# The last 64 rows of a product as 64-row matmuls, two f tiles side by side on the two parts of the array

## What is computed

```python
# attention: y of shape (B, H, S, D) -> x of shape (1536, 320)
h = x @ w_in                                  # 320 -> 2048
g = np.maximum(0.01 * h, h)
x = g @ w_out                                 # 2048 -> 320
expert_idx = np.argmax(x @ w_gate, axis=1)    # 8 experts, up to 384 tokens in each
h = np.maximum(np.einsum('ecd,edf->ecf', disp, w1), 0.0)   # 320 -> 1024, by expert
y = np.einsum('ecf,efd->ecd', h, w2)                       # 1024 -> 320
out[i] = gate_w[i] * y[expert_idx[i], pos[i]]
```

## Time and profile before

| | us |
|---|---|
| median of 3 runs | 449.36 |
| lowest to highest | 449.0 to 451.3 |
| the profiled execution, its own time | 448.94 |
| its span, from the first to the last instruction | 447.2 |
| PE busy in the span | 419.4 |
| DVE, ACT, POOL busy | 266.3, 218.2, 183.2 |
| mean granted TensorE clock, share of full speed | 0.979 |

### The profile page before, as it was taken

How to read it: one execution, slowest core, us unless ns; L and a number is a source line. 1 busy time by engine, 2 the same in 40 slices (tenths; PEclk the granted TensorE clock), 3 DMA queues, 4 the chain that set the end, 5 groups by cost and what they waited for, 6 DMA issues and landing times.

```text
span 447.2 us, 8125 instructions
## 1 busy us (share of the span) xinstructions
PE 419.4 (94%) x3025; PEld 397.9 (89%) x3025; DVE 266.3 (60%) x549; ACT 218.2 (49%) x484; POOL 183.2 (41%) x183
## 2 busy tenths in 40 slices
PE   7979999999999999999999999699999999999990
PEld 4958999899899989899999995399999999999990
DVE  6796786856479746388543643365663756755220
ACT  5616647463444354352443332156754677665431
POOL 3763525511121302010478000617474868881613
PEclk8999999999999999999999998989999999999996
DMA  8999704403221410000450404382875578760001
GB/s 230 340 321 351 265 1 135 134 12 92 89 65 70 134 54 2 1 1 1 139 173 12 132 11 161 107 256 74 251 215 156 133 243 262 206 191 2 3 11 52
DMA packets 24377, 56.88 MB, mean 127 GB/s; under 512 B 4868, under 2 KB 9670, under 8 KB 24332
## 3 DMA queue, kind: packets, MB, share of 16 engines
q1 hardware_dynamic: 19132, 47.88, 34.6%
q0 software_dynamic: 2688, 6.56, 5.3%
q10 hardware_dynamic: 2512, 1.82, 1.2%
HBM read 50.03 MB, written 8.31 MB: 130 GB/s over the span
## 4 chain that ended last, share of the span: by engine, by line
PE 80%; DVE 7%; ACT 5%; issue 4%; DMA 2%; POOL 1%; SPq 0%; DVEq 0%; POOLq 0%; ACTq 0%
PE bank L1261 20%; PE bank L1267 10%; PE bank L1248 9%; PE bank L1249 8%; PE bank L1250 8%; PE bank L1252 4%; PE bank L1251 4%; PE bank L1161 4%; PE bank L1114 2%; PE bank L1297 2%; PE bank L1338 2%; PE bank L1144 1%; ACT ee L629 1%; DMA nat<-in_nat 1%; PE bank L1130 1%
## 5 line engine op out<-in xcount | busy, mean ns | idle before, releaser
L1043 DVE SCALAR_TENSOR_TENSOR gl<-bank,gh 128x384 fp32r<-128x384 f32 x64 | 35.6, 557 | 61.1 <-ACT gh L748 52.2
L728 ACT ACTIVATE tt<-bank 128x384 f32<-128x384 f32 x64 | 31.3, 489 | 77.8 <-PE bank L1252 77.8
L1261 PE MATMUL bank<-woh,gh 128*128 128x320 f32 x192 | 59.3, 319 | 3.1 <-ACT gh L734 1.5
L508 POOL TENSOR_TENSOR w2l<-w2r,w2h 128x640 fp32r<-128x640 f32 x28 | 43.9, 1570 | 40.4 <-ACT w2h L610 40.2
L748 ACT ACTIVATE gh<-bank 128x384 fp32r<-128x384 f32 x64 | 31.5, 492 | 59.0 <-PE bank L1267 52.3
L1025 DVE TENSOR_TENSOR gl<-g,gh 128x384 fp32r<-128x384 f32 x64 | 40.6, 634 | 32.7 <-ACT gh L734 32.5
L1017 DVE TENSOR_TENSOR g<-bank,tt 128x384 f32<-128x384 f32 x64 | 35.3, 552 | 39.6 <-ACT tt L728 39.0
L1261 PE MATMUL bank<-wol,gh 128*128 128x320 f32 x192 | 57.2, 308 | 0.0
L734 ACT ACTIVATE gh<-g 128x384 fp32r<-128x384 f32 x64 | 33.4, 523 | 44.3 <-DVE g L1017 44.3
L1248 PE MATMUL bank<-xh,wih 128*128 128x384 f32 x128 | 46.2, 361 | 0.5 <-DVE xh L823 0.5
L498 POOL TENSOR_TENSOR y<-hs,rec 128x320 f32<-128x320 f32 x11 | 8.9, 812 | 91.8 <-DVE hs L877 80.9
(11 more groups left out here) (196 smaller groups left out, 1054.5 us busy)
## 6 DMA issues: line engine op xcount, KB each, us to landing
w1r<-in_w SPq DMA_DIRECT2D x32, 384.0 KB, 4.7
w2r<-in_w SPq DMA_DIRECT2D x32, 320.0 KB, 3.4
qkt<-in_qk SPq DMA_DIRECT2D x12, 416.0 KB
ee<-gsc SPq DMA_DIRECT2D x9, 512.0 KB, 5.9
nat<-in_nat SPq DMA_DIRECT2D x12, 372.0 KB, 5.0
wir<-in_w_in SPq DMA_DIRECT2D x4, 768.0 KB, 12.6
wor<-in_w_out SPq DMA_DIRECT2D x4, 640.0 KB, 14.5
nat<-in_nat SPq DMA_DIRECT2D x12, 160.0 KB, 4.9
```

The source lines that it names most:

```text
L508: gp.tensor_tensor(lo, raw, hi.bitcast(F32), ALU.subtract).then_inc(s_lo2, 1)
L728: a.activation(tt[m % 2][:], ps_h[m % 2][:, 0:TM], ACT.Copy, scale=0.01).then_inc(s_t, 1)
L1043: ve.scalar_tensor_tensor(gl[m % 2][:], ps_h[m % 2][:, 0:TM], 0.0, gh[m % 2][:].bitcast(F32), ALU.max, ALU.subtract).then_inc(s_gl, 1)
L1261: mm(ab, gh[m % 2][:, cols], w[:, f, c0:c1], start=first and f == 0 and i == 0, stop=False, skip_group_check=True)
```

## The change

`hidden` treats steps in pairs of an even and an odd f. The even step makes its first seven matmuls as before; the eighth, lo weights by x_hi, takes partitions 0 to 63 alone. Right behind it a 64-row matmul on partitions 64 to 127 makes the same part for f + 1, into the other bank, and opens that bank's sum. The odd step then has seven matmuls and goes on with a sum already begun. Since partitions 64 to 127 of x_hi's third tile hold the lo part, x's hi part is needed there a second time: ACT copies it into a new tile `xr` before DVE puts lo in its place, and DVE waits for that copy (`s_xr`). The even step waits, ahead of its seventh matmul, until the other bank has been read: for `s_g` in the first MLP, for `s_gl` in the experts. The odd step waits for nothing at its start. The router's steps are moved so that those that use the bank's upper columns fall on even f. The zeroed tile moves into the place of the last token tile's x_hi, whose first copy waits for the transfer that reads the zeros.

```diff
+        xr = [sb(f"xr{i}", [P, TM], F32R) for i in range(2)]
+        zeros, _ = at("zeros", [P, DM], F32, r_x + (NTM - 1) * per_tile)
...
+            def x_hi_again(dst, src, s, sem_n):
+                act.wait_ge(s_xh, sem_n)
+                cols = slice(s * P, (s + 1) * P)
+                a.activation(dst[P - DR:P, cols], src[P - DR:P, 2, cols].bitcast(F32), ACT.Copy).then_inc(s_xr, 1)
+
             def x_hi(n):
                 act.wait_ge(s_yT, n + 1)
+                if n == NCH - SUB:
+                    act.wait_ge(s_zero, 16)
...
+                x_hi_again(xr[n // SUB % 2], xh[n // SUB], n % SUB, n + 1)
...
+                x_hi_again(xr[e % 2], xeh[e % 2], s, NCH + e * SUB + s + 1)
...
-                    if t >= 0 and f in (3, 4, 5):
-                        copy_x2t(t, (f - 3,))
+                    if t >= 0 and f in (3, 5, 7):
+                        copy_x2t(t, ((f - 3) // 2,))
...
+                dve.wait_ge(s_xr, sem_n)
                 ve.tensor_tensor(dst_h[64:128, 2, cols], src3[64:128, 2, :], dst_h[64:128, 2, cols].bitcast(F32),
                                  ALU.subtract).then_inc(s_xl, 1)
...
-                    if t >= 0 and f in (5, 6, 7):
-                        take_logits(t, f - 5, ps_h[m % 2][:, TM:TM + E])
-                    if t >= 0 and f == 11:
+                    if t >= 0 and f in (6, 8, 10):
+                        take_logits(t, (f - 6) // 2, ps_h[m % 2][:, TM:TM + E])
+                    if t >= 0 and f == 12:
                         take_ranks(t, ps_h[m % 2][:, TM:TM + SUB * E])
...
-            def hidden(m, wh, wl, f, x_hi, x_lo, nt):
-                if m >= 2:
+            def hidden(m, wh, wl, f, x_hi, x_lo, x_again, nt):
+                ts = slice(0, max(nt, 2) * P)
+                hb, other = ps_h[m % 2][:, ts], ps_h[1 - m % 2][:, ts]
+                even = f % 2 == 0
+                if even and m >= 2:
                     pe.wait_ge(s_gl, m - 1)
-                ts = slice(0, max(nt, 2) * P)
-                hb = ps_h[m % 2][:, ts]
                 for kt in range(2):
-                    mm(hb, wh[:, f, kt, :], x_hi[:, kt, ts], start=kt == 0, stop=False)
+                    mm(hb, wh[:, f, kt, :], x_hi[:, kt, ts], start=even and kt == 0, stop=False)
                     mm(hb, wl[:, f, kt, :], x_hi[:, kt, ts], start=False, stop=False)
                     mm(hb, wh[:, f, kt, :], x_lo[:, kt, ts], start=False, stop=False)
-                mm(hb, wh[:, f, 2, :], x_hi[:, 2, ts], start=False, stop=False)
-                mm(hb, wl[:, f, 2, :], x_hi[:, 2, ts], start=False, stop=True).then_inc(s_h, 1)
-
+                if even:
+                    if 1 <= m <= M2:
+                        pe.wait_ge(s_g, m)
+                    elif m > M2:
+                        pe.wait_ge(s_gl, m)
+                    mm(hb, wh[:, f, 2, :], x_hi[:, 2, ts], start=False, stop=False)
+                    mm(hb, wl[0:DR, f, 2, :], x_hi[0:DR, 2, ts], start=False, stop=True).then_inc(s_h, 1)
+                    mm(other, wl[P - DR:P, f + 1, 2, :], x_again[P - DR:P, ts], start=True, stop=False)
+                else:
+                    mm(hb, wh[:, f, 2, :], x_hi[:, 2, ts], start=False, stop=True).then_inc(s_h, 1)
```

More of the change, by code:

```diff
@@ L55, in mlstm_moe_kernel @@
         base = ((nc.sbuf_base + 31) // 32) * 32
-        room = (nc.sbuf_usable_end - base) // 32 * 32 - 64
+        room = (nc.sbuf_usable_end - base) // 32 * 32 - 32
         ctx.enter_context(nc.sbuf_tensor("arena", [P, room], mybir.dt.uint8))
@@ L170, in mlstm_moe_kernel @@
         wg = sb("wg", [P, KT, E], F32)
-        zeros = sb("zeros", [P, DM], F32)
         before = sb("before", [P, P], BF16)
@@ L271, in mlstm_moe_kernel @@
         s_rec, s_z, s_y, s_yT = sem("recip"), sem("z_ready"), sem("y_ready"), sem("yT")
-        s_xh, s_xl = sem("x_hi"), sem("x_lo")
+        s_xh, s_xl, s_xr = sem("x_hi"), sem("x_lo"), sem("x_hi_last_rows_again")
         s_h, s_t, s_g, s_gh, s_gl, s_acc = sem("mlp_h"), sem("mlp_t"), sem("mlp_g"), sem("g_hi"), sem("g_lo"), sem("mlp_acc")
@@ L743, in _ @@
                         store(t)
-                    if t >= 0 and f == 9:
+                    if t >= 0 and f == 11:
                         router(t)
@@ L1030, in _ @@
                         attention(n, k)
-                    if t >= 0 and f == 8:
+                    if t >= 0 and f == 10:
                         router(t, lgs[:])
-                    if t >= 0 and f == 9:
+                    if t >= 0 and f == 11:
                         count(t)
-                    if t >= 0 and f == 10:
+                    if t >= 0 and f == 13:
                         gates_of(t)
-                    if t >= 0 and f == 11:
+                    if t >= 0 and f == 12:
                         places(t)
-                    if t >= 0 and f == 12:
+                    if t >= 0 and f == 14:
                         gate_parts(t)
@@ L1347, in h_step @@
                         pe.wait_ge(s_lo1, f // 2 + 1)
-                    hidden(m, wih, wil, f, xh[t], xl[t], nt)
+                    hidden(m, wih, wil, f, xh[t], xl[t], xr[t % 2], nt)
                 else:
@@ L1354, in h_step @@
                         pe.wait_ge(s_lo1, NPM + NPE * e + f // 2 + 1)
-                    hidden(m, ew[e % 3][0], ew[e % 3][1], f, xeh[e % 2], xel[e % 2], nt)
+                    hidden(m, ew[e % 3][0], ew[e % 3][1], f, xeh[e % 2], xel[e % 2], xr[e % 2], nt)
             def acc_step(m, nt):
@@ L1378, in _ @@
                 t, f = m // FI - 1, m % FI
-                if t >= 0 and f in (5, 6, 7, 11):
+                if t >= 0 and f in (6, 8, 10, 12):
                     pe.wait_ge(s_gl, m - 1)
-                    if f == 11:
+                    if f == 12:
                         positions(t, ps_h[m % 2][:, TM:TM + SUB * E])
                     else:
-                        logits(t, f - 5, ps_h[m % 2][:, TM:TM + E])
+                        logits(t, (f - 6) // 2, ps_h[m % 2][:, TM:TM + E])
                 h_step(m, SUB)
@@ L1392, in _ @@
                     acc_step(m - 1, SUB)
-                if t >= 0 and f in (3, 4, 5):
-                    transpose_x2(t, f - 3)
+                if t >= 0 and f in (3, 5, 7):
+                    transpose_x2(t, (f - 3) // 2)
                 for n, k in tasks_at(m, 1):
```

## The result

The changed kernel takes 485.41 us (median of 4, 483.2 to 492.3) beside 450.33 of the kernel before; the ratio is 1.078 with a 95% interval from 1.072 to 1.084. (Ratios in this document leave out executions more than 1.5% above the fastest of their kernel, here the one of 492.3.) Forecast were 485 and a range of 475 to 496. The profiled execution took 483.20 us, its span is 481.4.

What follows compares the result with a forecast made beforehand. PE was taken to bound the first MLP and the experts, without slack. 448.94 + 16.2 (mode, saving included) + 19.6 (wait) = 484.7; with the runs' median .4 above, 485 us, range 475 to 496.

Steps and rivals of the forecast that it cites:

- Part 1: First layer, both stages: one matmul slot saved per pair of steps, 7.2 + 2.7 = 9.9 us.
- Part 2: 64-row matmuls among full ones on PE: mode changes cost 16.2 us net, the saved matmuls already included.
- way in: PE, full to half height: .27 us from the last 384-column full matmul's start to the load.
- open load: PE weight load not hidden beside the previous matmul: .10 us entering half height, .11 leaving.
- way out: PE, half to full height: .27 us taken for 384 columns, bounds .27 and .32.
- Part 3: New wait before even steps' seventh matmul: 19.6 us lost in the experts, nothing put down for the first MLP.
- the restart: PE resuming after the new wait in the experts: .05 + .08 us for each of 29, 3.8 us.
- Part 4: ACT's extra copies, DVE's wait for them, the zeros' new place and moved router steps: put at nothing.
- halves one after another: Rival 1, each pair on PE: second half streams after the first, 9.9 us more, 495 us; chance 10%.
- the falling clock: Rival 2, experts: granted clock falls as PE idles, some 11 us more, 496 us; chance 9%.
- the free mode: Rival 3, PE's 64-row pairs: change of mode costs nothing, waits stay, 459 us; chance 5%.
- The fourth: Rival 4: packing free, and gl not late because gh begins relatively earlier, 439 us; chance 3%.

Runs made afterwards that it cites:

- the wait alone: Kernel before with only the new wait added ahead of the seventh matmul of each even step, all matmuls full height: 474.47 us, ratio 1.047.
- the run that forces it: Changed kernel with each pair's second half matmul on the same partitions 0 to 63 as the first: 494.88 us, ratio 1.101.
- the mode alone: Kernel before with the eighth matmul of every even step cut to partitions 0 to 63, no new wait, no matmul saved: 476.63 us, ratio 1.055.

## Why the prediction was right, step by step

**The bound.** PE bounds both stages; a wait put on PE cost its whole length (the wait alone: 23 us). The other half, that a matmul less is worth its whole slot in both, held in the experts alone.

**Part 1** was its weakest step. 9.9 us were put down for the saved matmuls, at a full slot each. Taken by itself, that saving shows in the experts (4.3 forecast, 5.5 measured by the medians), and in the first MLP by 3.7 us of 5.6 in one profile, without a gain in the medians. The total didn't suffer: with the mode's price paid in the same step, the first MLP's +7.4 is the forecast +7.5. That stretch also holds three waits for g, 1.1 us, which had been put at nothing.

**Part 2**, the mode. The scores' neighbourhood was the right place to look: way in .27 forecast and .27 measured, open load .10 and .10, halves within .01 and within .01, way out .27 taken (bounds .27 and .32) and .28 measured, open load .11 and .10. The drain that the Trainium skill names (TensorEngine Tiling, Key Properties) is in the rows at both ends of each pair; the packing rule holds too, but only inside the pair, and a pack of two saves .175 us (384 columns) against a price of .4.

**Part 3**, the wait. 19.6 us forecast for the experts, 19.3 measured by starts and records. Inside the sum errors cancel: the restart was put at .13 us and is .05 + .10; of the six steps behind a weight split, counted at .7 to 1.8 (one of them in the earlier trace rows), four stand at 1.2, one at 1.0 and one at .7; and three even steps that had a lag before have none after. The lag's origin, ACT's wait for the accumulate, was tested by a third buffer; the part of it that is DVE's own was taken to be smaller than it is. Not foreseen were four waits of .5 to 1.6 us, 3.6 in all, at the start of steps (the last three lines of waits above). All four are at f = 2, the first step after the jump to the next expert's code; the kernel before has two such waits with .6 us. They take the place of the three missing lags, and with them the experts come to +31.2 rather than +28.3.

What PE waits for there isn't what the view names. Step f = 2 asks for a weight split that is made an expert ahead, and for gl of two steps back. The longest of the four (timeline of after, and between its last two rows the instruction queue in 403.7 to 404.9 us):

```profile
384.70 0.96 DVE L827 TENSOR_TENSOR w1l<-w1r,w1h 128x768 fp32r<-128x768 f32 x1 [0.17 <-ACT w1h L607]
...
404.17 0.56 DVE L1055 SCALAR_TENSOR_TENSOR gl<-bank,gh 128x384 fp32r<-128x384 f32 x1 [2.46 <-ACT gh L759]
...
q8 instruction: 1, 0.02, 5.7%
...
406.86 0.36 PE L1263 MATMUL bank<-xeh,w1h 128*128 128x256 f32 x1 [1.61 <-DVE gl L1055]
```

The split asked for ends at 385.66 and the gl at 404.73, both long before 406.86; the other three stops are alike, with the split done 19 us or more before. But a 16 KB packet of the instruction queue ends at 404.88, 1.98 us before PE goes on, and two of the other three starts come 1.99 and 2.16 us after such a packet. In the traces of all runs, each wait at f = 2 of the second, fifth and sixth expert ends 1.9 to 2.3 us after one, 25 in all. So it is PE's code that comes late there, as far as traces can tell; no run tested it, and the stop in the first expert (297.67) doesn't fit.

**Part 4**, the rest at nothing: 1.003 with an interval that holds 1. The 1.4 us more of waits for ACT's gh in that profile aren't in the changed kernel, and whether the copies cause them isn't shown.

**The sum** came out within 0.4 us of the median, and that is partly luck: the profiled execution lost 3 us more in the experts than forecast and 4.4 less around them (first and third line of the table), and neither stretch holds anything that the change was meant to shorten. In the first the kernel before has a granted clock of .50 from 8.9 to 12.3 us, the changed kernel none. In the third PE waits for the first expert's tokens (DVE's xeh), 2.1 us before and .5 after. That one may not be chance: the stretch takes 23.7 to 24.4 us in the four kernels with pairs in the experts and 24.9 to 27.0 in the eight without, and why stays open. **The rivals**: halves one after another is ruled out by the run that forces it (+10 us), the falling clock by the granted clock of .99 in the experts, as before (one stretch at .50 in either, 292.2 to 295.6 us before, 408.7 to 412.1 after), the free mode by the mode alone (+25 us). The fourth, gh beginning earlier, didn't happen by itself; made to happen with a third buffer it still leaves 5.6% over the kernel before, mostly the mode's price.

## What to carry to other kernels

A half-height matmul among full ones pays twice for the change (here about .4 us, more than two slots of 384 columns): look for a place in the trace where both kinds already meet and read the distance of starts and the longer records there; by these numbers packing can pay only for runs of packed matmuls long enough to spread that price, which no run here tried. When a step opens the next step's accumulator early, the wait for that buffer moves forward by a step; lay the readers' times beside the new place in the trace of before, and count from start to start, since idle time in the waits' view is less than what is lost. The engine that a wait is put down to should be checked against the time when its result was ready: at f = 2 all that the step asks for had been ready for a microsecond or more.

## What the hardware showed beyond that

The granted clock of the first MLP isn't always 1.00: in some executions it falls to .50, the 1.2 GHz level, for some us, each time in tile 1 or 2 and shortly after one of PE's two .9 us waits before the scores. In the kernel with the wait alone (busy time by stretch):

```profile
116.00:119.90 3.90, 2.98 (x28) 2.76 (x28) 1.25 (x2) 0.91 (x3) 0.00 (x0) 1.00 0.00 0
119.90:123.30 3.40, 3.40 (x16) 3.40 (x15) 1.04 (x3) 1.01 (x2) 0.00 (x0) 0.50 0.02 5
123.30:126.00 2.70, 2.70 (x21) 2.65 (x20) 1.23 (x4) 0.49 (x1) 0.00 (x0) 1.00 0.00 0
```

There 16 matmuls are recorded in 3.4 us of full work, where the neighbours have 21 in 2.7. At half the clock such a stretch costs at most half its length, 1.7 us. This kernel has a second one, 184.7 to 188.1 us; six of the others have one or two. The waits alone don't decide it: the profiled executions before and after have the same two waits of .9 us and no such stretch. The clock goes with the differences between executions of one kernel: of the 13 of the kernel before that were run beside this one, the five with a mean granted clock of .959 to .971 took 454.3 to 455.0 us, the eight at .976 to .981 448.8 to 452.4.
